# Attention and two MLPs on one core: token sums one a step, an earlier place for the local scores, wide filler products, and a later load

## The chip, the cores and the metric

The program runs on one core of one Trainium2 chip, in fp32 (with fp32r products in the MLPs). The metric is the device time of one execution in microseconds (us). Engines are named as in the profile: PE (TensorE), DVE (VectorE), ACT (ScalarE), POOL (GpSimd) and SP (SyncE, which issues the DMAs).

## What is computed

```python
# q, k, v: (4, 8, 576, 64)
q_d, k_d, v_d = means of q, k, v over groups of 4 positions      # 144 positions
out_up  = repeat(softmax(q_d k_d^T / 8) v_d, 4)
out_loc = softmax(q k^T / 8 where |i - j| < 4) v
x = (out_up + out_loc) as (2304, 512)
x = ((x @ w1) * (x @ w2)) @ w3 @ w_out                           # d_ff 1024
h = x @ w_in;  out = (h * sigmoid(h)) @ w_out2                   # d_ff 2048
```

w3 @ w_out is folded into one matrix while attention runs.

## The kernel before

Attention handles 16 pairs of heads, one pair a **step** (`step(s)`, s = 0 to 15, written once on each engine), and step 16 finishes it. Every engine's order is written out by hand; engines meet in semaphores only. In step s PE does, in this order:

- `scores_down(s)` (L1148): scores of the pooled heads of pair s, read by ACT's exponentials `prob_d`;
- from step 4 on, half of `multiply(q)`, q = s - 4 (L1115): six of the twelve products of one sixteenth of w3 @ w_out; q is called a **half** below, since two of them make a block of 128 rows;
- `turn_local` (L1167) and `turn_down` (L1159): transposes of the probabilities of pair s - 1;
- the other half of `multiply(q)`;
- `scores_local(s+1)` (L1133): banded scores of the next pair, which DVE masks into `sc` (L761) and of which it takes the minimum `low` (L769), which ACT's exponentials (L510) wait for;
- `weighted_local` (L1190) and `weighted_down` (L1177): values of pair s - 1, which DVE adds into `x` (L803) in the step after.

The step of the first transposes is also where steps 1 to 3, which have no `multiply` yet, carry **fillers**: `warm(n)` (L1123) issues products with the identity whose results nobody reads, n by the table `FILL` = (before scores_down, before turn_down, after turn_down).

After every odd q, ACT (L447) and DVE (L735) take the finished bank of w3 @ w_out into `r2` as a high and a low part, at the end of that step; the next q waits for DVE's part. Steps 5, 7, 9, 11, 13 and 15 have such a taking, so steps 6, 8, 10, 12, 14 and 16 have the wait.

DVE's step is: `x` of pair s - 2, maximum of the pooled scores (L775), pooling of the next pair (L749, `qkd`), totals of the exponentials and their inverse (L782 to L788, `inv`), then token sums if the table `TOKENS` has some for the step, then `sc` and `low` of the next pair, the taking of `r2`, and the pooled totals. A **token sum** (L712) is one 128x768 difference of blocks of x, four of them (`tr`), which the first MLP stage reads as one of the operands of a seven-product scheme for 2x2 blocks. POOL multiplies `prob` by `inv` (L424) and takes low parts of w3 (L393).

SP issues the loads in one list: for t = 0 to 15 in the order v (pooled), w3, q and k, v (windows), each with a wait on the engine that frees its buffer. w_out comes in two loads of 1 MB, `load_w_out(0)` and `(1)`; DVE and ACT split them in steps 1 to 5 by `W_OUT`, blocks 4 to 7 (the later half) in steps 3 and 4 on ACT.

After attention come 48 sets of MLP products (L1035, L1064, L1093), which the change does not touch.

Of the kernel before, what the change touches and what calls it, by code (L numbers as in the profile page):

```python
# [12 lines left out]
P = 128  # L13
BANK = 512
# [3 lines left out]
def attention_then_mlps(nc, dims, qk_in, vg_in, vw_in, w3_in, w_out_in, sets_in, w_out2_in, out):  # L18
# [8 lines left out]
    PAIRS = B * HP  # L27
# [58 lines left out]
    with ctx:  # L86
# [3 lines left out]
        def sem(name):  # L90
# [3 lines left out]
        ident = sb("ident", [P, P])  # L94
# [61 lines left out]
        ps = ctx.enter_context(nc.psum_tensor("ps", [P, 8, BANK], F32))  # L156
        pS, pD, pP, pO, pW = 0, 2, 4, 6, 7
# [55 lines left out]


        SUMS = (8, 12)
        TOKENS = {14: (0,), 15: (1, 2, 3)}


        FILL = {1: (30, 4, 2), 2: (6, 6, 2), 3: (6, 6, 2)}
        EXTRA = {8: ("weights", 0), 10: ("tokens", 0), 11: ("weights", 1), 12: ("tokens", 1), 13: ("tokens", 2),  # L220
                 14: ("tokens", 3)}

        def halves_of(s):

# [42 lines left out]
        def _(sp):  # L267
# [47 lines left out]
            for t in range(PAIRS):  # L315
                if t == 1:
                    load_w_out(0)
                    load_qk(3)
                if t + 1 < PAIRS:
                    load_vg(t + 1)  # L320
                if t >= FOLD - 2:
                    load_w3(t - FOLD + 2)
                if t == 1:
                    load_w_out(1)
                if t > 0 and t + 3 < PAIRS:
                    load_qk(t + 3)
                if t + 1 < PAIRS:
                    load_vw(t + 1)
                if t + 2 in SUMS:
                    load_weights(SUMS.index(t + 2))  # L330
# [680 lines left out]
        def _(pe):  # L1011
# [107 lines left out]

            def warm(n):  # L1120

                for _ in range(n):
                    nc.tensor.transpose(ps[:, pW, 0:P], ident[:, :], ident[:, :])  # L1123

            def scores_local(s):
                pe.wait_ge(qk_here[s % 3], 16 * (s // 3) + 16)
# [12 lines left out]
            def step(s):  # L1139
                u, w = s % 2, (s - 1) % 2  # L1140

                def scores_down():
                    pe.wait_ge(pooled, s + 1)
                    after(pe, exp_d, s)
                    for g in range(2):
                        for h in range(2):
                            rows = slice(h * D, (h + 1) * D)
                            e = nc.tensor.matmul(ps[0:PD, pD + h, g * SD:(g + 1) * SD],  # L1148
                                                 qkd[rows, u, 0, g * PD:(g + 1) * PD], qkd[rows, u, 1, :],
                                                 start=True, stop=True)  # L1150
                    e.then_inc(scored, 1)
# [42 lines left out]

                qs = halves_of(s)
                if s == PAIRS:
                    for part in range(2):
                        multiply(qs[0], part)
                    turn_local()
                    turn_down()  # L1200
                    for part in range(2, 4):
                        multiply(qs[0], part)
                    for part in range(2):
                        multiply(qs[1], part)
                    weighted_local()
                    weighted_down()
                    for part in range(2, 4):
                        multiply(qs[1], part)
                    for q in qs[2:]:
                        for part in range(4):  # L1210
                            multiply(q, part)
                    return

                warm(FILL[s][0] if s in FILL else 0)
                scores_down()
                for part in range(2):
                    for q in qs:
                        multiply(q, part)
# [5 lines left out]
                for part in range(2, 4):  # L1224
                    for q in qs:
                        multiply(q, part)
                if s + 1 < PAIRS:
                    scores_local(s + 1)
                if s > 0:
                    weighted_local()  # L1230
                    weighted_down()

            warm(9)
            scores_local(0)
            for s in range(PAIRS + 1):
                step(s)
# [83 lines left out]
```

## Time and profile before

| | us |
|---|---|
| median of 3 runs (lowest, highest) | 804.48 (803.36, 804.74) |
| the profiled execution's own time | 805.16 |
| its span, first to last instruction | 803.3 |
| attention, to the end of the last L1115 | 139.66 |
| PE busy over the span | 783.5 |

The span begins at the first instruction; times in the rows count from there. Attention is the part up to 139.66 us; all that the change touches lies in it.

### The profile page before, as it was taken

The page shows a single profiled execution, that of the slowest core. Times are in us where ns is not written, and L with a number is a line of the kernel's source. Part 1 is how long each engine was busy: PE and PEld are TensorE (multiplying, and loading weights), DVE is VectorE, ACT ScalarE, POOL GpSimd, SP SyncE. Part 2 cuts the span into 40 slices and gives each one's busy share as a digit, 9 for nine tenths or more (in the row PEclk, how much of TensorE's full clock was granted, in tenths as well). Part 3 has the DMA queues.
Part 4 walks back from the last instruction along what each step waited for, and adds up shares of the span by engine and source line. Part 5 has one row for each costly group of instructions (what it writes and reads, how often), then busy time and mean ns, then how long its engine had stood idle before and what let it go on. Part 6 is the DMA issues. An engine that isn't in the chain of part 4 may idle for free.

```text
span 803.3 us, 13951 instructions
## 1 busy us (share of the span) xinstructions
PE 783.5 (98%) x5433; PEld 702.0 (87%) x5433; DVE 587.7 (73%) x939; ACT 347.6 (43%) x791; POOL 272.7 (34%) x305
## 2 busy tenths in 40 slices
PE   7899998999999999999999999999999999999998
PEld 6677776899998999999999888898889888988987
DVE  7887788776678676677778676779677679756644
ACT  6788886422443324332264233254233344433321
POOL 7878985522331331332213221114132113212100
PEclk9899999999999999999999999999999999999999
DMA  9757731111011011011122211223121122312102
GB/s 323 245 184 242 242 125 53 54 53 52 28 53 51 29 53 53 27 53 52 48 84 75 84 53 53 78 80 131 56 101 54 53 79 76 134 53 94 39 1 78
DMA packets 23040, 69.83 MB, mean 87 GB/s; under 512 B 2496, under 2 KB 2496, under 8 KB 22976
## 3 DMA queue, kind: packets, MB, share of 16 engines
q1 hardware_dynamic: 22976, 68.95, 25.5%
q8 instruction: 43, 0.70, 0.3%
q14 instruction: 21, 0.17, 0.1%
HBM read 64.23 MB, written 4.72 MB: 86 GB/s over the span
## 4 chain that ended last, share of the span: by engine, by line
PE 90%; DVE 5%; ACT 3%; issue 1%; DMA 0%; DVEq 0%; ACTq 0%
PE ps L1035 44%; PE ps L1093 25%; PE ps L1064 13%; PE ps L1115 5%; ACT prob L510 1%; DVE sc L761 1%; DVE low L769 1%; PE ps L1133 1%; PE ps L1167 1%; PE ps L1177 1%; PE ps L1190 1%; DVE tr L712 1%; PE ps L1159 1%; DVE qkd L749 0%; PE ps L1148 0%
## 5 line engine op out<-in xcount | busy, mean ns | idle before, releaser
L1035 PE MATMUL ps<-xb,wa 128*128 128x384 f32 x2016 | 404.9, 338 | 0.4 <-DVE mu L863 0.2
L1035 PEld LDWEIGHTS ps<-xb,wa 128*128 128x128 f32 x2016 | 355.1, 188 | 22.4 <-DVE mu L863 1.4
L381 POOL TENSOR_TENSOR rw<-rw 128x256 f32<-128x256 f32 x192 | 170.2, 907 | 448.8 <-DMA rw<-in_sets 336.7
L863 DVE TENSOR_TENSOR mu<-ps,mu 128x384 f32<-128x384 f32 x132 | 73.2, 554 | 123.5 <-PE ps L1035 123.2
L1064 PE MATMUL ps<-g,r 128*128 128x512 f32 (+1 forms) x576 | 124.9, 338 | 2.1 <-issue 2.1
L612 ACT ACTIVATE a<-a 128x384 f32<-128x384 f32 x72 | 37.9, 526 | 187.3 <-DVE a L863 187.3
L1093 PE MATMUL ps<-w2h_even,g 128*128 128x512 f32 x432 | 113.2, 394 | 0.0
L1093 PE MATMUL ps<-w2h_odd,g 128*128 128x512 f32 x432 | 112.5, 393 | 0.0
L718 DVE TENSOR_TENSOR wa<-rw,wa 128x1024 fp32r<-128x1024 f32 x96 | 107.0, 1115 | 3.5 <-ACT wa L447 3.4
L1064 PEld LDWEIGHTS ps<-g,r 128*128 128x128 f32 x576 | 97.7, 188 | 10.6 <-issue 2.6
L1093 PEld LDWEIGHTS ps<-w2h_odd,g 128*128 128x128 f32 x432 | 79.9, 188 | 11.9
L1093 PEld LDWEIGHTS ps<-w2h_even,g 128*128 128x128 f32 x432 | 79.8, 188 | 11.7
L863 DVE TENSOR_TENSOR a<-ps,mu 128x384 f32<-128x384 f32 x108 | 59.9, 555 | 36.6 <-PE ps L1035 35.5
L447 ACT ACTIVATE wa<-rw 128x1792 fp32r<-128x1792 f32 (+2 forms) x49 | 81.4, 1663 | 0.0
L447 ACT ACTIVATE mu<-ps 128x384 f32<-128x384 f32 x48 | 23.4, 487 | 103.5 <-PE ps L1035 103.5
L890 DVE TENSOR_TENSOR g<-a,g 128x384 fp32r<-128x384 f32 x96 | 63.7, 664 | 3.3
L447 ACT ACTIVATE g<-a 128x384 fp32r<-128x384 f32 x48 | 25.2, 526 | 81.8 <-DVE a L869 65.0
L1115 PE MATMUL ps<-r,w3t 128*128 128x512 f32 x192 | 53.4, 418 | 5.9 <-DVE r L735 5.6
L1115 PEld LDWEIGHTS ps<-r,w3t 128*128 128x128 f32 x192 | 35.2, 195 | 15.7 <-issue 8.8
L888 DVE CAST g<-a 128x384 fp32r<-128x384 f32 x96 | 43.7, 455 | 0.0
L510 ACT ACTIVATE prob<-sc,low 128x64 f32<-128x64 f32 x96 | 32.1, 338 | 7.1 <-DVE low L769 6.9
L875 DVE TENSOR_TENSOR g<-a,g 128x384 fp32r<-128x384 f32 x48 | 33.1, 692 | 0.5
(78 smaller groups left out, 705.2 us busy)
## 6 DMA issues: line engine op xcount, KB each, us to landing
rw<-in_sets SPq DMA_DIRECT2D x48, 512.0 KB, 3.5
w2r<-in_w_out SPq DMA_DIRECT2D x24, 512.0 KB, 3.5
qk<-in_qk SPq DMA_DIRECT2D x16, 576.0 KB, 6.6
vg<-in_vg SPq DMA_DIRECT2D x16, 336.0 KB, 4.9
vw<-in_vw SPq DMA_DIRECT2D x16, 320.0 KB, 3.1
out<-osb SPq DMA_DIRECT2D x18, 256.0 KB, 2.5
wn<-in_w SPq DMA_DIRECT2D x16, 256.0 KB, 4.6
raw<-in_w_out SPq DMA_DIRECT2D x2, 1024.0 KB, 12.7
```

The lines of the kernel that those rows point to most:

```text
L381: nc.gpsimd.tensor_tensor(blocks[:, o, :], blocks[:, a, :], blocks[:, b, :], op).then_inc(done, 1)
L447: return nc.scalar.activation(o, a, ACT.Copy)
L510: e = nc.scalar.activation(prob[:, u, g, 1 - h, :], sc[:, g, h, :], ACT.Exp, bias=low[:, u, n:n + 1], scale=-1.0, accum_out=tot[:, u, to, ...
L612: nc.scalar.activation(q, q, ACT.Silu).then_inc(g_act, 1)
L718: e = nc.vector.tensor_tensor(wa[:, k % 2, 1, blocks, :], rw[:, k % 2, 1 + blocks.start:1 + blocks.stop, :], wa[:, k % 2, 0, blocks, :].bi ...
L863: nc.vector.tensor_tensor(o, half_bank(k, i), term, ALU.add).then_inc(sum_ready, 1)
L888: nc.vector.tensor_copy(g[:, 0, j % 2, q // 2, to], a4[:, q, :]).then_inc(g_hi, 1)
L890: nc.vector.tensor_tensor(g[:, 1, j % 2, q // 2, to], a4[:, q, :], g[:, 0, j % 2, q // 2, to].bitcast(F32), ALU.subtract).then_inc(g_lo, 1)
L1035: e = nc.tensor.matmul(ps[:, (k + i) % 2, 0:TH], wa[:, k % 2, l, A_SLOT[i], a * P:(a + 1) * P], xb[:, i, r, a, :], start=(i in (0, 1, 4) a ...
L1064: e = nc.tensor.matmul(o, r2[:, m + MT // 2 * f, l, b * P:(b + 1) * P], g[:, r, n % 2, f, to], start=(first and p == 0 and not (rest and b ...
L1093: e = nc.tensor.matmul(ps[:, 2 + tb, :], g[:, l, j % 2, q // 2, at], w2h[j % 2][:, q // 2, r, :], start=(c == 0 and a < 2 and p == 0), sto ...
L1115: e = nc.tensor.matmul(ps[:, fold_bank(q), :], w3t[:, l, a, :], r3[:, a, r, :], start=(a == 0 and p == 0), stop=(a == MT - 1 and p == 2))
```

## The change

Five edits. The token sums are spread over steps 11 to 14. In steps 5 to 14 `scores_local(s+1)` is issued right behind `scores_down(s)`. `warm(n)` issues plain products of up to 512 columns in place of transposes of 128, and its counts are halved. The later half of w_out is loaded one round of SP's list later. In step 16 the third quarter of q = 12 comes ahead of the transposes. (The table `EXTRA` was read by nothing.)

```diff
--- before.py
+++ after.py
@@ -213,12 +213,10 @@
 
 
         SUMS = (8, 12)
-        TOKENS = {14: (0,), 15: (1, 2, 3)}
-
-
-        FILL = {1: (30, 4, 2), 2: (6, 6, 2), 3: (6, 6, 2)}
-        EXTRA = {8: ("weights", 0), 10: ("tokens", 0), 11: ("weights", 1), 12: ("tokens", 1), 13: ("tokens", 2),
-                 14: ("tokens", 3)}
+        TOKENS = {11: (0,), 12: (1,), 13: (2,), 14: (3,)}
+
+
+        FILL = {1: (15, 2, 1), 2: (3, 3, 1), 3: (3, 3, 1)}
 
         def halves_of(s):
 
@@ -320,7 +318,7 @@
                     load_vg(t + 1)
                 if t >= FOLD - 2:
                     load_w3(t - FOLD + 2)
-                if t == 1:
+                if t == 2:
                     load_w_out(1)
                 if t > 0 and t + 3 < PAIRS:
                     load_qk(t + 3)
@@ -1119,8 +1117,11 @@
 
             def warm(n):
 
-                for _ in range(n):
-                    nc.tensor.transpose(ps[:, pW, 0:P], ident[:, :], ident[:, :])
+                while n > 0:
+                    m = min(n, BANK // P)
+                    nc.tensor.matmul(ps[:, pW, 0:m * P].rearrange("p (m c) -> p m c", m=m), ident[:, :],
+                                     ident[:, None, :].broadcast_to([P, m, P]), start=True, stop=True)
+                    n -= m
 
             def scores_local(s):
                 pe.wait_ge(qk_here[s % 3], 16 * (s // 3) + 16)
@@ -1194,12 +1195,11 @@
 
                 qs = halves_of(s)
                 if s == PAIRS:
-                    for part in range(2):
+                    for part in range(3):
                         multiply(qs[0], part)
                     turn_local()
                     turn_down()
-                    for part in range(2, 4):
-                        multiply(qs[0], part)
+                    multiply(qs[0], 3)
                     for part in range(2):
                         multiply(qs[1], part)
                     weighted_local()
@@ -1213,6 +1213,9 @@
 
                 warm(FILL[s][0] if s in FILL else 0)
                 scores_down()
+                soon = s > FOLD and s + 1 < PAIRS
+                if soon:
+                    scores_local(s + 1)
                 for part in range(2):
                     for q in qs:
                         multiply(q, part)
@@ -1224,13 +1227,13 @@
                 for part in range(2, 4):
                     for q in qs:
                         multiply(q, part)
-                if s + 1 < PAIRS:
+                if s + 1 < PAIRS and not soon:
                     scores_local(s + 1)
                 if s > 0:
                     weighted_local()
                     weighted_down()
 
-            warm(9)
+            warm(4)
             scores_local(0)
             for s in range(PAIRS + 1):
                 step(s)
```

PE in step 5, before. L1148 is scores_down, L1115 multiply, L1167 and L1159 the transposes, L1133 scores_local; the count is of instructions as written, each plain fp32 one of which the trace shows as two.

```order
L1148 MATMUL ps<-qkd 72x144 x4
L1115 MATMUL ps<-r,w3t 128x512 x6
L1167 MATMUL ps<-ident,prob 128x128 x5
L1159 MATMUL ps<-ident,prob_d 112x72 x6
L1115 MATMUL ps<-r,w3t 128x512 x6
L1133 MATMUL ps<-qk 64x64 x20
```

The same place now; lines have moved by up to three, L1134 is scores_local.

```order
L1149 MATMUL ps<-qkd 72x144 x4
L1134 MATMUL ps<-qk 64x64 x20
L1113 MATMUL ps<-r,w3t 128x512 x6
L1168 MATMUL ps<-ident,prob 128x128 x5
L1160 MATMUL ps<-ident,prob_d 112x72 x6
L1113 MATMUL ps<-r,w3t 128x512 x6
```

The twenty local scores have moved ahead of all twelve products of multiply and of the transposes.

DVE in step 15, before, from the pooled maximum on.

```order
L775 TENSOR_REDUCE lowd<-ps 72x2x2
L782 TENSOR_REDUCE tot<-prob 128x4
L786 TENSOR_REDUCE tot<-tot 128x10
L788 RECIPROCAL inv<-tot 128x10
L712 TENSOR_TENSOR tr<-x,tr 128x768
L712 TENSOR_TENSOR tr<-x 128x768
L712 TENSOR_TENSOR tr<-x,tr 128x768
L735 TENSOR_TENSOR r<-ps,r 128x512
```

DVE in step 12 now, where one of them has gone.

```order
L773 TENSOR_REDUCE lowd<-ps 72x2x2
L747 TENSOR_REDUCE qkd<-qk 128x288
L780 TENSOR_REDUCE tot<-prob 128x4
L784 TENSOR_REDUCE tot<-tot 128x10
L786 RECIPROCAL inv<-tot 128x10
L710 TENSOR_TENSOR tr<-x,tr 128x768
L759 SCALAR_TENSOR_TENSOR sc<-ps,mask 128x5x64 x2
L767 TENSOR_REDUCE low<-sc 128x10
```

Three sums have left the way of L735 in step 15, and each of steps 11 to 14 has one ahead of the masking.

PE's first entries, before, to the first turn of the probabilities.

```order
L1123 MATMUL ps<-ident 128x128 x9
L1133 MATMUL ps<-qk 64x64 x20
L1148 MATMUL ps<-qkd 72x144 x4
L1133 MATMUL ps<-qk 64x64 x20
L1123 MATMUL ps<-ident 128x128 x30
```

And now.

```order
L1122 MATMUL ps<-ident 128x512
L1134 MATMUL ps<-qk 64x64 x20
L1149 MATMUL ps<-qkd 72x144 x4
L1134 MATMUL ps<-qk 64x64 x20
L1122 MATMUL ps<-ident 128x512 x3
L1122 MATMUL ps<-ident 128x384
```

Over steps 0 to 3, 73 transposes have become 13 plain products, of about half as many columns in all.

## Rows read from the trace of the kernel before

**Rows 1.** The page: busy time of each engine, its share of the span, instructions.

```profile
PE 783.5 (98%) x5433; PEld 702.0 (87%) x5433; DVE 587.7 (73%) x939; ACT 347.6 (43%) x791; POOL 272.7 (34%) x305
```

**Rows 2.** Stretches of attention: busy us and operations by engine, PE clock, DMA.

```profile
29.60:32.40 2.80, 0.07 (x2) 0.00 (x0) 2.32 (x7) 1.20 (x8) 1.92 (x2) 1.00 0.38 131
32.40:39.60 7.20, 7.18 (x36) 5.30 (x35) 5.22 (x12) 4.95 (x19) 6.12 (x6) 0.53 0.66 214
43.30:86.30 43.00, 41.27 (x718) 31.81 (x716) 35.69 (x78) 37.86 (x167) 37.65 (x39) 1.00 0.69 227
86.30:114.40 28.10, 27.23 (x478) 21.22 (x476) 23.53 (x52) 24.65 (x110) 24.57 (x26) 1.00 0.61 197
...
124.00:128.30 4.30, 4.27 (x18) 3.70 (x19) 4.30 (x6) 1.07 (x3) 4.06 (x4) 0.60 0.13 33
```

**Rows 3.** What PE waited for, 0 to 140 us: total, times, longest.

```profile
PE ps L1115 <- DVE r L735: 5.6, 6, 3.3
PE ps L1190 <- issue: 2.7, 1, 2.7
```

**Rows 4.** Timeline around the pause: start, us, engine, operation, idle before it.

```profile
28.77 0.90 PE L1190 MATMUL ps<-pt,vw 64*64 64x57 f32 x38 [0.18 <-ACT pt L447]
...
32.42 0.27 PE L1190 MATMUL ps<-pt,vw 64*64 64x58 f32 x2 [2.75 <-issue]
...
34.35 0.82 DVE L803 TENSOR_TENSOR x<-ps,od 128x344 f32<-128x344 f32 x2 [1.45 <-ACT od L522]
...
41.98 0.89 DVE L761 SCALAR_TENSOR_TENSOR sc<-ps,mask 128x320 f32<-128x320 f32 x2 [2.72 <-PE ps L1133]
```

**Rows 5.** DMA queues, 29.6 to 31 us: packets, MB, share of 16 engines.

```profile
q8 instruction: 1, 0.02, 4.7%
```

**Rows 6.** The page: instruction queue over the whole span: packets, MB, share.

```profile
q8 instruction: 43, 0.70, 0.3%
```

**Rows 7.** Timeline of PE at step 1, with the first fillers.

```profile
7.61 3.49 PE L1123 MATMUL ps<-ident 128*128 128x128 f32 x30
11.84 0.43 PE L1148 MATMUL ps<-qkd 64*72 64x144 f32 x3 [0.73 <-ACT prob_d L498]
```

**Rows 8.** Timeline of PE, DVE and ACT in steps 13 and 14.

```profile
100.36 0.71 PE L1148 MATMUL ps<-qkd 64*72 64x144 f32 x8
...
104.95 0.81 PE L1133 MATMUL ps<-qk 64*64 64x64 f32 x40
...
105.83 0.89 DVE L761 SCALAR_TENSOR_TENSOR sc<-ps,mask 128x320 f32<-128x320 f32 x2 [1.29 <-PE ps L1133]
...
106.36 0.59 ACT L447 ACTIVATE r<-ps 128x512 fp32r<-128x512 f32 x1
...
107.17 0.71 PE L1148 MATMUL ps<-qkd 64*72 64x144 f32 x8
...
107.49 0.68 DVE L735 TENSOR_TENSOR r<-ps,r 128x512 fp32r<-128x512 f32 x1
...
108.32 1.63 PE L1115 MATMUL ps<-r,w3t 128*128 128x512 f32 x6 [0.43 <-DVE r L735]
```

**Rows 9.** Timeline of step 15 and 16: token sums (L712), POOL, the wait.

```profile
111.86 1.63 DVE L712 TENSOR_TENSOR tr<-x 128x768 f32<-128x768 f32 x1
...
118.48 0.93 DVE L712 TENSOR_TENSOR tr<-x,tr 128x768 f32<-128x768 f32 x1
...
118.67 1.87 POOL L393 TENSOR_TENSOR w3t<-wn,w3t 128x512 fp32r<-128x512 f32 x1
...
119.14 0.60 ACT L447 ACTIVATE r<-ps 128x512 fp32r<-128x512 f32 x1
119.33 2.02 DVE L712 TENSOR_TENSOR tr<-x 128x768 f32<-128x768 f32 x1
...
121.28 2.01 DVE L712 TENSOR_TENSOR tr<-x,tr 128x768 f32<-128x768 f32 x1
...
124.03 2.18 PE L1115 MATMUL ps<-r,w3t 128*128 128x512 f32 x6 [3.30 <-DVE r L735]
```

## The prediction

> **What bounds the kernel now.** I read the page first: PE is busy for 783.5 us, 98% of the span [rows 1], so a change gains by ending PE's waits or a low clock, or by taking work off PE. Then the waits of PE alone in attention. Two kinds stand out: 5.6 us in six waits of L1115 for DVE's `r` (L735), the longest 3.3, and one of 2.75 put down to "issue", that is to nothing that the profile shows [rows 3]. Then the table by stretches, for what such a wait costs afterwards: behind both long idles the granted clock is low, 0.53 over 7.2 us and 0.60 over 4.3 us, where the stretches around have 1.00 [rows 2]; the lower level is 1.2 GHz, the full one 2.4. PE is busy all through these two stretches, so they cost 7.2 x 0.47 = 3.4 and 4.3 x 0.40 = 1.7 us of PE time. Of PE's attention time, then, 2.75 + 3.4 = 6.1 us hang on the pause in step 3, and 3.3 + 1.7 = 5.0 us on the wait for `r` in step 16. Last the timeline of one pair of steps: step 13 goes from 100.36 to 107.17, 6.81 us with no wait in it, and step 14 begins with 0.43 us of idle PE ahead of L1115 [rows 8]. PE's own work of a step is therefore 6.81 us, and what is over that is a wait.
>
> **The change, part by part.**
>
> *Token sums.* In step 15 three sums stand ahead of L735 on DVE. They run from 118.48 to 123.29 [rows 9], 4.8 us. Without them DVE takes `r` as soon as ACT has written its part, at 119.14 + 0.60; with 0.68 for L735 [rows 8] that is 120.4, before PE is through with step 15 at 124.03 - 3.30 = 120.7 [rows 9]. The next operands in the way of PE would be the pair's normalised probabilities: POOL's L424 stood behind one 1.87 us L393 [rows 9], 0.6 of it waiting for a sum, and what follows on POOL comes earlier too; I find them ready in time (an estimate, from the same durations without the stops), with the third quarter of q = 12 put ahead of the transposes (three more products, 0.7 us of cover). So the 3.3 us and the low clock behind it both go: **-5.0 us**.
>
> What do the sums cost where they go? A sum takes 0.93 us alone and 1.63, 2.02 and 2.01 in the other three cases [rows 9]. The third began at 119.33 while POOL's L393 ran until 120.54, and ended 0.81 after that: it stood still until POOL was done. The second ran while L393, begun at 118.67, waited, and took 1.87 for it. One of the two engines stops for the other's whole operation. The Trainium skill says this too (SBUF — State Buffer, Who interferes with whom): a DVE instruction with two SBUF inputs and a GpSimd one that reads SBUF exclude each other, and the second blocks fully; this trace agrees in these rows, and by that rule the moved sums would each tend to the long price, since POOL's L393 and L424 stand at that place in every step. I take 1.3 us as a mean, bounds 0.93 and 2.02. DVE is busy 23.53 us in steps 11 to 14, one sum of 1.63 included [rows 2], so 21.9 without; with four sums 25.6 to 30.0, at 1.3 each 27.1, against 4 x 6.81 = 27.2 of PE. DVE comes close to bound in these four steps and no more, because the earlier scores end DVE's idle 1.29 us ahead of `sc` [rows 8]. PE feels a lag only when `r` is later than the two score blocks that now precede L1115, 1.4 us into a step. I put 0.3 us on steps 11 to 14 for it (bounds 0 and 2.8, the upper from 30.0 - 27.2).
>
> *Local scores earlier.* L1115 of an even step waits for `r`, which waited for ACT at 106.36 + 0.59 and for `sc`, `low` on DVE (105.83 on), which waited for the scores [rows 8]. Now `sc` no longer waits for PE at all, and the scores (L1133, 0.81 us, some 0.75 without overlap [rows 8]) run between scores_down and L1115. ACT's part alone puts `r` at 106.95 + 0.68 = 107.6, and PE wants it at 107.17 + 0.65 + 0.75 = 108.57: the 0.43 us wait is covered. Steps 5 to 10 last 43.0 us [rows 2] against 6 x 6.81 = 40.9, 2.1 over; in step 5 DVE also has w_out's split (L818) and I leave 0.5 of it standing in step 6: **-1.6**. Steps 11 to 15 last 34.4 (86.3 [rows 2] to 120.7) against 4 x 6.81 + 6.1 = 33.3, where step 15 is 6.81 less the scores it does not have. That is -1.1, with the 0.3 above **-0.8**. Nothing is queued badly behind the moved wait: it is for q and k, which land a step earlier, and for `sc` of the pair before, which DVE does in the previous step; if DVE lags by more than a microsecond, scores_local itself will wait there, which is the same lag, not another.
>
> *Fillers.* Thirty transposes take 3.49 us, and PE then still waits 0.73 us for ACT's exponentials [rows 7]. No plain fp32 product of 512 columns is in the trace. Bounds per column and trace entry: 0.62 ns (scores_down, 0.71 us for 8 entries of 144 [rows 8]) and 0.91 ns (a transpose, 3.49 us for 30 of 128 [rows 7]); two entries a product and 1,920 columns give 2.4 to 3.5 us. I take 3.5, since a full 128x128 array is what the transposes have too and the scores not. PE then arrives as before. At 2.4 it would be idle 1.8 us, still under the 2.75 that came ahead of a fallen clock. No time by itself: **0**.
>
> *What the fewer fillers do to the pause.* The pause of 2.75 us falls inside L1190, between its 38th and 39th entry of 40 [rows 4], where the code has no wait. The page has an instruction queue with 43 packets of 16 KB, for 5,433 products and as many weight loads: one block per 253 entries [rows 1, 6]. One of its packets moves between 29.6 and 31 us [rows 5], in the middle of the pause. So I read the pause as PE out of instructions: the block was asked for when the one before was begun, and lay behind data loads. By the counts of the timeline PE had passed 470 products, 940 entries, at the pause. The 73 transposes before it become 26 entries of products (13 of two each), 94 entries fewer with their weight loads; the same block end is now reached in step 4 rather than in step 3, some 5 us later, and its request comes when the queues are nearer to empty (they run low from 30 us on: 38% busy, 131 GB/s in the pause's stretch [rows 2]). The load of w_out that is moved back, 1 MB, leaves the queue ahead of it as long as before at 27 us, and shorter before. It is issued about a step later, and ACT splits it first at the end of step 3, after the pause's place. The Trainium skill (Runtime: NRT & Kernel Launch, Instruction fetch mechanics) has blocks of 256 instructions, fetched through a queue of their own while the current one runs; the rows' 253 agree. It also gives PE room for 2,048 instructions, by which 940 entries could not run dry, and the pause would be of another kind and stay, 797.1: a part of the first rival.
>
> PE gets back up to 6.1 us, but the other engines don't all follow. DVE was idle 1.45 + 2.72 = 4.2 us between the pause and step 5 [rows 4], so its chain can move up by at most 4.2, and it bounds PE at `r` in step 6. POOL and ACT are full in step 4. I take **-3.3** (bounds 0 and -4.2).
>
> *Sum:* -5.0 - 1.6 - 0.8 - 3.3 = -10.7. The rows belong to an execution of 805.16, so 794.5; the median is 0.7 below that execution, so **794.0**. What follows attention moves up whole: its loads and sums wait for PE and DVE's own progress.
>
> **The rivals.**
>
> *The pause stays, or another takes its place.* For it: the request of each block still falls among loads, in steps 5 to 10 the DMA engines are 69% busy [rows 2], and with shorter steps a block has less time; the new place is in step 4. Against: 94 entries are a third of a block, and no later block paused. The gain is then 7.4: 797.1; with a pause in a worse place (the whole 6.1 instead of 3.3), 799.5. Of its chance of 0.2, 0.05 is for a pause that is no lack of instructions and stays at its place.
>
> *DVE becomes the bound in steps 11 to 14.* If every sum takes 2.0, DVE has 30 us of work for 27.2. For it: POOL is 87% busy there (24.57 of 28.1 [rows 2]). Against: POOL's long operations were in the way of three sums in four only, and one engine's stop is then the other's gain. Costs 2.5: 796.5. Chance 0.12.
>
> *Slower.* The one way that I see is that instructions run short again and again: the request now falls just behind SP's batch of loads in every step from 5 on. Each pause costs up to 6.1, so two more than before, with the old one kept, give 7.4 - 12.2 = 4.8 slower, 809; from a second one on it decides. Against it: the waits have a single "issue" entry in all of attention [rows 3], though every step of 5 to 15 used about one block. Chance 0.03.
>
> *The edits do little.* If PE's wait in step 16 is taken over by POOL's L424 and L415, only half of the 5.0 comes back, and with the pause kept too the result is 800 to 803. Chance 0.05.
>
> My forecast has 0.6. Its own range is 792 to 796 (3.3 between 1.5 and 4.2, 0.3 up to 1.5). To leave out no more than 2 in 10 the range takes in the first two rivals: **791 to 799**. Of this kernel a difference below 0.2% (1.6 us) can't be told from none. Faster by more 0.94, within 0.03, slower 0.03.
>
> **What would show it.** The idle of L1115 for `r` near 120 us is gone and the clock stays at 1.00 there; L1115 waits less than 0.3 us in every even step from 8 on; `sc` never waits for PE from step 6 on; the "issue" pause in step 3 is absent, and the clock holds from step 1 to the end of attention; steps 7 to 10 last 6.8 us each; the last L1115 ends near 129 (139.66 before). I am wrong if a pause of over 2 us stands anywhere on PE in attention, if L1115 or scores_local waits for DVE in steps 12 and 14 by more than a microsecond, or if the first scores_down waits longer than before and the clock falls in step 1.

## The result: 798.86 us, faster, with half of the gain that was forecast

| | before | after |
|---|---|---|
| median of 6 runs | 804.54 us (803.36 to 804.90) | 798.86 us (798.22 to 801.34) |
| after / before | | 0.9935, 95% interval 0.9922 to 0.9948 |
| span of the profiled execution | 803.3 us | 796.9 us |
| last L1115 (L1113 after) ends | 139.66 us | 133.07 us |

The kernel is faster by 5.7 us in the medians, and by 5.2 (4.2 to 6.3) by the ratio, which takes in all runs. The forecast was 10.5. The direction was right and the time lies inside the range by 0.1 us, but the gain is about half of what the sum gave. All of the difference lies in attention: from there to the end the two executions take 663.6 and 663.8 us.

The page of the changed kernel, against [rows 1, 6]; the products fell by 47, the 43 blocks of instructions stayed:

```profile
PE 783.3 (98%) x5386; PEld 695.9 (87%) x5386; DVE 591.7 (74%) x939; ACT 347.0 (44%) x791; POOL 272.7 (34%) x305
...
q8 instruction: 43, 0.70, 0.3%
```

What PE waited for between 0 and 142 us (total, times, longest), against [rows 3]:

```profile
PE ps L1113 <- issue: 1.0, 1, 1.0
PE ps L1113 <- DVE w3t L739: 0.7, 1, 0.7
...
PE ps L1113 <- DVE r L733: 0.5, 1, 0.5
PE ps L1113 <- DVE r L816: 0.5, 1, 0.5
```

The two long idles of before are gone: `r` costs 0.5 where it cost 5.6, and there is no "issue" of 2.7 in L1190. Two waits are new, 1.0 and 0.7 us on L1113; the wait of L1168 (L1167 before) for `x` is 1.4 in all where it was 0.6. The stretches (columns as in [rows 2]):

```profile
10.00:30.00 20.00, 18.81 (x340) 12.75 (x338) 18.72 (x39) 18.89 (x87) 16.50 (x17) 1.00 1.01 326
30.00:133.00 103.00, 99.02 (x1504) 74.99 (x1501) 91.11 (x177) 87.46 (x358) 87.56 (x85) 1.00 0.58 184
...
38.92:82.08 43.16, 42.16 (x716) 32.33 (x714) 37.38 (x82) 37.98 (x167) 38.86 (x41) 1.00 0.70 227
82.08:116.80 34.72, 34.49 (x558) 26.22 (x556) 30.97 (x61) 30.34 (x135) 31.84 (x31) 1.00 0.56 176
116.80:133.10 16.30, 14.64 (x111) 11.10 (x110) 14.58 (x17) 11.35 (x23) 9.66 (x8) 1.00 0.22 66
```

The granted clock (third column from the right) is 1.00 in all of attention behind 10 us. In steps 5 to 10 (third row) PE is idle for 1.0 of 43.16 us, in steps 11 to 15 for 0.23, and still these steps are as long as before (43.0 and 34.4). So PE is busy longer with the same products. One step of the timeline shows with what, against [rows 8] (start, us, engine, operation):

```profile
96.01 0.71 PE L1149 MATMUL ps<-qkd 64*72 64x144 f32 x8
96.66 0.81 PE L1134 MATMUL ps<-qk 64*64 64x64 f32 x40
97.40 1.66 PE L1113 MATMUL ps<-r,w3t 128*128 128x512 f32 x6
...
101.34 0.91 PE L1191 MATMUL ps<-pt,vw 64*64 64x57 f32 x40
102.18 0.86 PE L1178 MATMUL ps<-ptd,vd 96*64 96x144 f32 x8
102.97 0.71 PE L1149 MATMUL ps<-qkd 64*72 64x144 f32 x8
```

From start to start scores_local (L1134) takes 0.74 us and weighted_local (L1191) 0.84; before, where they stood behind each other, they took 0.63 and 0.80. From step 7 to step 13 every step lasts 6.96 us, with no wait in it. It remains to look at step 16, PE and DVE:

```profile
122.01 1.48 DVE L716 TENSOR_TENSOR wa<-rw,wa 128x768 fp32r<-128x768 f32 x1
...
123.42 1.48 DVE L728 TENSOR_TENSOR xb<-x,xb 128x768 fp32r<-128x768 f32 x1
...
124.82 1.50 DVE L739 TENSOR_TENSOR w3t<-wn,w3t 128x512 fp32r<-128x512 f32 x1
126.23 1.77 DVE L728 TENSOR_TENSOR xb<-tr,xb 128x768 fp32r<-128x768 f32 x1
126.41 3.00 PE L1113 MATMUL ps<-r,w3t 128*128 128x512 f32 x12 [1.00 <-issue]
127.92 0.81 DVE L801 TENSOR_TENSOR x<-ps,od 128x344 f32<-128x344 f32 x2
128.65 0.68 DVE L733 TENSOR_TENSOR r<-ps,r 128x512 fp32r<-128x512 f32 x1
129.25 0.68 DVE L739 TENSOR_TENSOR w3t<-wn,w3t 128x512 fp32r<-128x512 f32 x1
130.07 3.00 PE L1113 MATMUL ps<-r,w3t 128*128 128x512 f32 x12 [0.66 <-DVE w3t L739]
```

Both new waits end with an L739, the conversion of the low part of w3 on DVE. The first is printed as "issue", but PE goes on 0.09 us after the L739 that began at 124.82 is through. In front of the first, DVE works on L716 and L728, parts that the MLP will need; in front of the second on another L728, on `x` (L801) and on `r` (L733).

The stretches against the forecast's:

| stretch | forecast | measured |
|---|---|---|
| to the start of step 5 (43.32 before, 38.92 after) | -3.3 | -4.4 |
| steps 5 to 10 (43.0 before, 43.16 after) | -1.6 | +0.2 |
| steps 11 to 15 (34.4 before, 34.72 after) | -0.8 | +0.3 |
| step 16, from where PE is ready (120.7 before, 116.80 after) to its last product | -5.0 | -2.7 |

### The profile page after: what moved, and what is told of

The parts are those of the page before. It is cut to its first block, busy times and chain, and to the rows that moved or that the text cites. A ratio compares the mean times of both kernels' runs of the same rounds, so it can differ in the third digit from the quotient of the medians.

```text
span 796.9 us, 13857 instructions
## 1 busy us (share of the span) xinstructions
PE 783.3 (98%) x5386; PEld 695.9 (87%) x5386; DVE 591.7 (74%) x939; ACT 347.0 (44%) x791; POOL 272.7 (34%) x305
## 4 chain that ended last, share of the span: by engine, by line
PE 88%; DVE 9%; ACT 1%; issue 1%; DMA 0%; POOL 0%; DVEq 0%; ACTq 0%
PE ps L1033 44%; PE ps L1091 25%; PE ps L1062 13%; PE ps L1113 2%; DVE qkd L747 1%; DVE sc L759 1%; DVE r L816 1%; DVE low L767 1%; PE ps L1134 1%; DVE tr L710 1%; DVE x L801 1%; PE ps L1191 1%; PE ps L1178 1%; DVE lowd L773 1%; PE ps L1149 0%
## 5 line engine op out<-in xcount | busy, mean ns | idle before, releaser
L716 DVE TENSOR_TENSOR wa<-rw,wa 128x1024 fp32r<-128x1024 f32 x96 | 107.1, 1116 | 3.8 <-ACT wa L445 3.5
L1062 PEld LDWEIGHTS ps<-g,r 128*128 128x128 f32 x576 | 97.8, 188 | 10.5 <-issue 2.6
L1113 PE MATMUL ps<-r,w3t 128*128 128x512 f32 x192 | 52.1, 408 | 2.7 <-issue 1.0
L1113 PEld LDWEIGHTS ps<-r,w3t 128*128 128x128 f32 x192 | 33.7, 188 | 11.3 <-issue 4.0
```

Source lines behind the costliest of these rows:

```text
L716: e = nc.vector.tensor_tensor(wa[:, k % 2, 1, blocks, :], rw[:, k % 2, 1 + blocks.start:1 + blocks.stop, :], wa[:, k % 2, 0, blocks, :].bi ...
L1062: e = nc.tensor.matmul(o, r2[:, m + MT // 2 * f, l, b * P:(b + 1) * P], g[:, r, n % 2, f, to], start=(first and p == 0 and not (rest and b ...
L1113: e = nc.tensor.matmul(ps[:, fold_bank(q), :], w3t[:, l, a, :], r3[:, a, r, :], start=(a == 0 and p == 0), stop=(a == MT - 1 and p == 2))
```

## The experiments

Each is compared with the kernel before on the same chip, whose medians were 804.5, 804.6, 805.8 and 804.7 us on the four chips. Where a run is compared with the changed kernel, that is its median of 798.86 from the result, unless the text says otherwise; what is said of waits and steps comes from one profiled execution of each. Names with b_ are the kernel before with one edit done, names with a_ the changed kernel with one edit undone or altered.

### One edit at a time

**b_fill**: before, with the wide fillers and their counts.

```diff
-        FILL = {1: (30, 4, 2), 2: (6, 6, 2), 3: (6, 6, 2)}
+        FILL = {1: (15, 2, 1), 2: (3, 3, 1), 3: (3, 3, 1)}
...
-                for _ in range(n):
-                    nc.tensor.transpose(ps[:, pW, 0:P], ident[:, :], ident[:, :])
+                while n > 0:
+                    m = min(n, BANK // P)
...
-            warm(9)
+            warm(4)
```

> The kernel before with the wide fillers and their halved counts alone. Theory 1 (the pause in step 3 is PE out of instructions, and 94 entries fewer move the block's end to a later place): the pause of 2.75 us is gone and with it the low clock behind it; the chain through DVE lets 3 to 4 us of it reach the end, 801 us against 804.5. Theory 2 (the pause belongs to its place or to the load of w_out): it stays in L1190 of step 3 and the time is within 0.5 us of before. Both: the wait for r in step 16 stays, 3.3 us, with a low clock behind it.

802.98 us, ratio 0.9977 (0.9966 to 0.9989): 1.5 faster. There is no pause in step 3 any more, and step 5 begins at 38.99 against 43.32. The first theory held for the pause, but not for the time, 801. In the profiled execution the gain is 3.2 us at the start of step 7 (54.87 against 58.10) and 2.5 at the end of attention: the wait for `r` stays at 3.3, and the clock behind it is low for longer than in [rows 2]:

```profile
119.00:125.80 6.80, 5.03 (x19) 4.28 (x20) 6.77 (x9) 2.64 (x5) 4.95 (x6) 0.50 0.20 70
```

**b_tokens**: before, with the new places of the token sums alone.

```diff
-        TOKENS = {14: (0,), 15: (1, 2, 3)}
+        TOKENS = {11: (0,), 12: (1,), 13: (2,), 14: (3,)}
```

> The kernel before with the token sums in steps 11 to 14 alone. Theory 1 (step 16 is bound by DVE's queue of low parts once the 3.3 us wait is gone): PE's wait for r goes, about 1 to 1.7 us of new waits for L741 come in its place, the clock stays full; 2.5 to 3.5 us faster than before, 801.5. Theory 2 (the whole 5.0 comes back and the shortfall of the changed kernel is elsewhere): 799.5. The pause in step 3 stays in both.

803.46 us, ratio 0.9984 (0.9971 to 0.9996): 1.0 faster. The wait of 3.3 is gone and no clock falls behind step 15, but step 14 now lasts 8.11 us instead of 7.28:

```profile
105.93 1.92 DVE L712 TENSOR_TENSOR tr<-x 128x768 f32<-128x768 f32 x1
...
109.41 0.68 DVE L735 TENSOR_TENSOR r<-ps,r 128x512 fp32r<-128x512 f32 x1
110.24 1.63 PE L1115 MATMUL ps<-r,w3t 128*128 128x512 f32 x6 [1.27 <-DVE r L735]
```

A sum stands in front of `sc`, `low` and `r` on DVE, and `sc` had no slack, since its scores came late. L741, the same line as L739 above, costs 0.7 and "issue" 0.5 in step 16 here too. The time is above what either theory gave.

**b_soon**: before, with the early local scores alone.

```diff
+                soon = s > FOLD and s + 1 < PAIRS
+                if soon:
+                    scores_local(s + 1)
...
-                if s + 1 < PAIRS:
+                if s + 1 < PAIRS and not soon:
```

> The kernel before with the early local scores in steps 5 to 14 alone. Theory 1 (0.43 us of wait saved in five steps, 0.15 us lost in ten): steps of 6.96 us each from 7 on, no wait for r in even steps, in all 0.5 to 1.2 us faster, 803.6, with the pause in step 3 and the wait in step 16 as before. Theory 2 (as forecast, steps of 6.81): 802.4.

803.83 us, ratio 0.9987 (0.9974 to 0.9999). From the start of step 5 to that of step 15 it needs 69.90 us where before needs 71.13. The waits for `r` of even steps are gone, and from step 7 on every step lasts 6.96.

Singly the three gain 1.5 + 1.0 + 0.8 = 3.3 us in the medians, and 4.2 by the ratios, each with an interval of some 1 us to both sides; all five edits together gain 5.7, and 5.2 by the ratio. These sums alone don't show that the edits help each other. The steps do: step 14 lasts 8.11 us with the moved sums alone and 7.13 with the early scores beside them. What a term is worth is therefore read below from the kernel with the others in place. The later load and the order of step 16 were not tried alone in the kernel before.

### One edit undone

**a_tokold**: changed, with the token sums at their old places.

```diff
-        TOKENS = {11: (0,), 12: (1,), 13: (2,), 14: (3,)}
+        TOKENS = {14: (0,), 15: (1, 2, 3)}
```

> The changed kernel with the token sums where they were (one in step 14, three in step 15), all else as changed. Theory 1 (moving them is worth the 3.3 us wait and part of the low clock, less 1.7 us of new waits for low parts of w3 in step 16 and less 0.4 of lag in steps 11 to 15): a wait of 3 us or more for r ahead of step 16, a low clock behind it, and 2.5 to 3.5 us over the changed kernel, 801.8. Theory 2 (the sums' move is worth its full 5.0 and the loss is in other edits): 803.8.

802.21 us, ratio 0.9974 (0.9959 to 0.9989): 3.4 slower than the changed kernel. The profiled execution is the fastest of the seven (800.58), and in it attention ends 1.9 later (134.93). The wait and the low clock are back, and the waits for L739 are not there:

```profile
119.34 3.89 PE L1113 MATMUL ps<-r,w3t 128*128 128x512 f32 x9 [3.11 <-DVE r L733]
...
127.83 7.10 PE L1113 MATMUL ps<-r,w3t 128*128 128x512 f32 x30
```

**a_late**: changed, without the early scores.

```diff
-                soon = s > FOLD and s + 1 < PAIRS
+                soon = False
```

> The changed kernel with scores_local(s + 1) behind the multiplies in every step again, so without the early local scores; all else as changed. Theory A, the term of my forecast (-1.6 in steps 5 to 10 and -0.8 in steps 11 to 15): 798.9 + 2.4 = 801.3; steps 7 to 11 alternate between 6.81 and 7.28 us instead of 6.96, and in steps 11 to 14, where DVE has the token sums and would stop again for the scores, they last 7.3 or more. Theory B: early scores gain only what they gained alone (804.6 to 803.8, 0.8 us), since each early block costs PE 0.15 us in the weighted_local that now stands behind a 512-column product: 799.7. Above 800.5 A, below 800.2 B.

801.24 us, ratio 0.995 (0.9933 to 0.9968): 2.4 slower (2.6 against a_quarter on the same chip, which is no different from the changed kernel). L1113 has five waits for `r`, 3.2 us in all, steps 7 to 10 alternate between 6.8 and 7.3, and step 14 takes 8.10 as in b_tokens. Step 15 begins at 112.16 instead of 110.10. My term of 2.4 holds, though alone the edit gains 0.8: it is the slack that it gives DVE that lets the token sums stand in steps 11 to 14.

**a_narrow**: changed, with the filler transposes and counts of before (the diff of b_fill the other way).

> The changed kernel with the transposes of before as fillers (73, and the old counts), all else as changed. Theory 1 (entry count decides): a pause of 2 to 3 us is back in step 3 near the 940th entry, the clock falls behind it, and the time is 3 to 4 us over the changed kernel, 802.5. Theory 2 (the later load of w_out removed the pause): no pause, time as the changed kernel, 798.9.

799.96 us, ratio 0.9936 (0.9921 to 0.9951). **a_wout**: changed, with the later half of w_out at its old place.

```diff
-                if t == 2:
+                if t == 1:
                     load_w_out(1)
```

> The changed kernel with the later half of w_out loaded where it was before, all else as changed. Theory 1 (the fillers alone moved the pause, the load's place is nearly free): within 0.5 us of the changed kernel, no pause. Theory 2 (the load decides): a pause of over 1 us and 3 to 4 us more, 802.5.

799.12 us, ratio 0.993 (0.9913 to 0.9946). Both times can't be told from the changed kernel's, and neither profile has the pause. My reading had put all of it on the count of fillers, and that fell here: with the old count and the later load there is no pause either. In a_wout a wait of 2.0 us for x in step 3 had half the clock behind it, for 3.4 us:

```profile
27.70:31.10 3.40, 3.40 (x23) 2.45 (x24) 3.40 (x4) 2.79 (x11) 3.24 (x4) 0.50 0.82 245
```

**a_both**: changed, with both of these edits undone; beside it **a_anchor**, the changed kernel as it is.

> The changed kernel with both early edits undone: the narrow filler transposes with their old counts, and the later half of w_out at its old place (t == 1). So token sums, early local scores and the order of step 16 alone. Theory (a shortage of instructions that needs both the old entry count and that load in the way, since either edit undone alone showed no pause): the pause is back in step 3, after the 472nd product, 2 to 4 us long, and the clock is low behind it. The end of attention in the profile is then 3 to 4.5 us later than in the changed kernel, as my term of -3.3 says: 801.5 to 803. Rival: the term is worth what the wide fillers gained alone, 1.5 us, since the engines behind PE give part of the pause back: 800.4.

> The changed kernel as it is, on the same chip as the run beside it, since the median of the kernel before was 1.2 us higher in one call than in the others. If that was the chip, the changed kernel comes out 5.7 us under its kernel before, between 798 and 800, with the two waits for w3_low (1.00 and 0.66 us) in step 16.

a_anchor 798.72 us (0.9921, 0.9904 to 0.9938); a_both 801.27 (799.83 to 803.16; 0.9954, 0.9937 to 0.9972), 2.6 slower. (On this chip the changed kernel gains 6.0 us in the medians.) The pause is back at its place, between the 38th and the 39th product. The profiled execution is the fastest of the seven and shows a short one, of 1.77 us, with no low clock behind it:

```profile
29.63 0.87 PE L1188 MATMUL ps<-pt,vw 64*64 64x58 f32 x38
32.27 0.27 PE L1188 MATMUL ps<-pt,vw 64*64 64x58 f32 x2 [1.77 <-issue]
```

A second, of 1.3 us, stands in step 4 on L1175. So, in these four kernels, the pause needs the old count of entries and that load in the queue.

### What the pause is

**b_shift**: before, with two more fillers at the very start.

```diff
-            warm(9)
+            warm(11)
```

> The kernel before with two more filler transposes at the very start (warm(11) for warm(9)): with their weight loads four trace entries more ahead of everything. Theory (a block of the program's code arrives late, and PE has run out of instructions): the pause of 2.7 us stays in step 3 but falls two products earlier in weighted_local, between its 36th and 37th entry instead of the 38th and 39th, at the same count of entries from the start; about 805. Rival (a wait or a port in weighted_local itself, or a place in the code): the pause stays between the 38th and 39th, or is somewhere else.

```profile
29.85 0.75 PE L1190 MATMUL ps<-pt,vw 64*64 64x58 f32 x36
32.49 0.33 PE L1190 MATMUL ps<-pt,vw 64*64 64x58 f32 x4 [1.89 <-issue]
...
50.01 0.71 PE L1148 MATMUL ps<-qkd 64*72 64x144 f32 x8 [0.69 <-issue]
```

Two more products at the start, and the pause falls two products earlier in a block of 40 that has no wait in it. The stretches up to the two idles (PE's count is the first in brackets):

```profile
0.00:32.00 32.00, 24.57 (x472) 20.61 (x473) 25.50 (x47) 23.69 (x106) 23.00 (x37) 1.00 0.92 307
0.00:49.60 49.60, 41.37 (x722) 33.04 (x722) 41.72 (x78) 37.92 (x166) 37.48 (x50) 0.97 0.79 261
```

It is 472 products in the kernel before too, and in b_tokens, b_soon and a_both. The second idle comes 250 products later, 500 entries with their weight loads, which is two blocks by the 253 of [rows 1, 6]. So a pause is bound to a count of instructions, not to a place in the work. (One execution, 804.0 us.) The 944 entries themselves are no whole number of such blocks; instructions that the trace doesn't count would have to make up the rest.

The traces show more than that: when the instruction queue's one packet moves ahead of each pause, and when PE goes on (us, read to 0.05).

| kernel | packet moves | PE goes on | between |
|---|---|---|---|
| before | 29.85 | 32.42 | 2.6 |
| b_tokens | 30.80 | 33.21 | 2.4 |
| b_soon | 31.75 | 34.26 | 2.5 |
| b_shift | 29.80, 47.60 | 32.49, 50.01 | 2.7, 2.4 |
| a_both | 29.90, 38.50 | 32.27, 41.01 | 2.4, 2.5 |

PE goes on 2.4 to 2.7 us behind the packet in all seven, whether it has stood still for 0.7 us or for 3.7. That fits a lack of instructions. It also says why one edit is enough. In a_both PE is through with its 472nd product at 30.50; the packet moves at 29.90, and 2.4 us behind it is 32.3, too late by 1.8. In a_narrow, with the later load, PE is as far at about the same time, but the packet has moved at 26.00. In a_wout, with fewer entries, the packet moves at 29.85 as before, but PE gets to its 472nd product only behind 37.98. That the load of w_out is what holds the packet up by those 4 us is argued from this one pair.

### Step 16 and the length of a step

**a_w3**: changed, with DVE's order in step 16 altered; the token parts and the last x are moved behind the conversions of w3.

```diff
+            w3_low(HALVES - 2)
             tokens_low(0, 0)
-            w3_low(HALVES - 2)
+            take_w3o(MT - 2)
+            w3_low(HALVES - 1)
             tokens_low(0, 1)
             take_local(PAIRS - 1)
-            take_w3o(MT - 2)
-            w3_low(HALVES - 1)
```

> The changed kernel with DVE's order in step 16 turned so that the low parts of the last two halves of w3 (L739) come ahead of the token parts (L728) and of the last x. Theory 1 (PE's two waits of 1.0 and 0.66 us there are DVE's queue): both go, 1.2 to 1.7 us faster than the changed kernel, 797.4. Theory 2 (the halves wait for the load of w3 or for ACT, or the products behind wait for the token parts instead): waits of the same sum stand there or at L1033, and the time is within 0.4 us of 798.9.

797.87 us, ratio 0.9913 (0.9899 to 0.9927), 1.0 faster than the changed kernel in the median of four runs, with intervals that overlap; the profile is what shows the effect. PE has no wait at all in step 16, and the last 30 products run in one piece:

```profile
125.07 7.15 PE L1113 MATMUL ps<-r,w3t 128*128 128x512 f32 x30
```

Behind the waits they took 1.66 + 3.00 + 3.00 = 7.66 us in three pieces: each stop cost, beside its own length, 0.25 us. I take that for a pipeline that ran empty, which was not tried. Step 16 goes from 118.11 to 132.22, 14.1 us against 16.3, so 2.2 back. The median shows 1.0 of it; in this profiled execution 1.3 was lost earlier, for another reason (last section). Step 16 begins 1.3 us later here than in the changed kernel, but that is not why the waits are gone: in a_wout and a_both it begins at 118.12, and both waits are there, 1.00 and 0.65 to 0.68 us.

**a_even**: changed, with early scores in even steps only.

```diff
-                soon = s > FOLD and s + 1 < PAIRS
+                soon = s > FOLD and s % 2 == 0 and s + 1 < PAIRS
```

> The changed kernel with the local scores behind the pooled ones in even steps only (6, 8, 10, 12, 14), in odd ones at their old place. Theory 1 (the early place costs 0.15 us in every step, since the weighted sums then stand behind a product of another shape instead of behind the scores): odd steps last 6.82, even ones 6.96 us or little more, 0.5 to 0.9 us faster, 798.2. Theory 2 (the 0.15 us is DVE's or ACT's lag): odd steps stay at 6.96 or grow, since the scores of the next pair come later again, and the time is 0.5 us or more above 798.9.

799.74 us, ratio 0.9939 (0.9925 to 0.9953), no gain. But it puts both orders side by side in one kernel, step 7 with the scores behind the multiplies and step 8 with them ahead:

```profile
58.88 0.81 PE L1134 MATMUL ps<-qk 64*64 64x64 f32 x40
59.52 0.87 PE L1191 MATMUL ps<-pt,vw 64*64 64x58 f32 x40
60.32 0.86 PE L1178 MATMUL ps<-ptd,vd 96*64 96x144 f32 x8
...
61.75 0.81 PE L1134 MATMUL ps<-qk 64*64 64x64 f32 x40
62.49 1.65 PE L1113 MATMUL ps<-r,w3t 128*128 128x512 f32 x6
...
66.44 0.91 PE L1191 MATMUL ps<-pt,vw 64*64 64x57 f32 x40
67.28 0.86 PE L1178 MATMUL ps<-ptd,vd 96*64 96x144 f32 x8
```

Behind each other the two blocks of 40 take 60.32 - 58.88 = 1.44 us. Apart they take 0.74 + 0.84 = 1.58. Steps 7 to 12 alternate between 6.81 and 6.96. From step 7 on this had won 0.47 us by the start of step 13 (95.61 against 96.01, from 54.30 against 54.23), and by step 15 it was gone, which begins at 110.32 (110.10 in the changed kernel): steps 13 and 14 last 7.20 and 7.51.

**a_best**: a_w3 with the scores early in even steps up to 10 and in all from 11 on.

```diff
-                soon = s > FOLD and s + 1 < PAIRS
+                soon = s > FOLD and (s % 2 == 0 or s > 10) and s + 1 < PAIRS
```

> The changed kernel with w3_low of the last two halves ahead of the token parts and of the last x on DVE in step 16 (as in the run that has only this), and the local scores early in even steps up to 10, and in every step from 11 on. Theory: in odd steps 5, 7 and 9 the scores stay behind the multiplies, weighted_local then takes 0.69 and not 0.84 us, and those steps last 6.81 us instead of 6.96; 3 x 0.15 = 0.45 below the run with the order in step 16 alone, 797.4, with steps 12 and 14 at 6.96 and no wait of PE for DVE in step 16. Rival: DVE bounds these steps, since it would stop for PE in odd steps, and what PE saves is waited off in step 11 or 12: 797.9, no different.

798.09 us, ratio 0.991 (0.9893 to 0.9926): no different from a_w3, and again without a wait in step 16. Step 14 lasts 7.58, with 0.59 us of L1113 waiting for `r`. The rival held: what PE saves, it waits off behind DVE.

**a_quarter**: changed, with the third quarter of the first multiply of step 16 behind the transposes again.

```diff
-                    for part in range(3):
+                    for part in range(2):
                         multiply(qs[0], part)
                     turn_local()
                     turn_down()
-                    multiply(qs[0], 3)
+                    for part in range(2, 4):
+                        multiply(qs[0], part)
```

> The changed kernel with the third quarter of the first multiply of step 16 behind the two transposes again. My forecast counted three products, 0.7 us, as cover for the turned local probabilities. Theory A: the cover is needed, turn_local waits for x or for POOL and ACT 0.5 to 0.7 us in step 16: 799.4. Theory B: nothing is late there, PE's waits in step 16 are for w3_low (L739) only, and they stay 1.66 us: 798.9, no different.

798.65 us, ratio 0.9922 (0.9906 to 0.9938), the same as the anchor's. The cover that I had counted was not needed: of the two waits of step 16 the one put down to "issue" is 0.5 long, the one for L739 0.7 as before.

## Why the forecast was half right

**Right.** The bound, PE's two long idles and the clock behind them; both went, and the clock holds to the end of attention. The pause as a lack of instructions, a reading that b_shift and the packets bear out: the 472nd product is its place whatever stands there. By the Trainium skill (Runtime: NRT & Kernel Launch, Instruction fetch mechanics) blocks of 256 are fetched ahead, and PE has room for 2,048. The blocks agree with the trace, 500 entries for two. No use of such a room shows: PE stood still at its 944th entry, for a packet that had moved 2.6 us before. The price of the fillers: 3.5 us was forecast for those of step 1, and a_anchor takes 3.49 (the profile of the changed kernel 4.18, see Open). The early scores: `sc` never waits for PE, and the term of 2.4 was 2.4 with the other edits in place. The price of the token sums, mean 1.3 us between 0.93 and 2.02, came out so:

```profile
86.03 0.94 DVE L710 TENSOR_TENSOR tr<-x 128x768 f32<-128x768 f32 x1
93.24 1.63 DVE L710 TENSOR_TENSOR tr<-x,tr 128x768 f32<-128x768 f32 x1
100.21 1.94 DVE L710 TENSOR_TENSOR tr<-x 128x768 f32<-128x768 f32 x1
108.09 1.63 DVE L710 TENSOR_TENSOR tr<-x,tr 128x768 f32<-128x768 f32 x1
```

Their mean is 1.5, and PE was not kept back until the last: step 14 lasts 7.13, and behind the sum at 108.09 `low` begins at 110.55, so that ACT's exponentials come late and step 15 takes 6.70 us. With the sums at their old places (a_tokold) it takes 6.29.

**The step that failed: "So the 3.3 us and the low clock behind it both go: -5.0".** They go, but not the whole time comes back: what is late now is w3_low (L739, L741 before) of the last two halves. I had followed the chain of `r` and POOL's L424, and no further down DVE's queue. In the kernel before the conversion for q = 14 was ready at 131.72, and PE wanted it at about 134.1, 1.5 us into its last thirty products:

```profile
123.21 0.68 DVE L735 TENSOR_TENSOR r<-ps,r 128x512 fp32r<-128x512 f32 x1
...
131.04 0.68 DVE L741 TENSOR_TENSOR w3t<-wn,w3t 128x512 fp32r<-128x512 f32 x1
...
132.56 7.10 PE L1115 MATMUL ps<-r,w3t 128*128 128x512 f32 x30
```

From the end of `r` (123.89) that is 7.8 us for DVE and 10.2 for PE, 2.3 to spare. In the changed kernel `r` ends at 116.60. DVE needs 9.7 us from there (to 126.32), and PE wants the same conversion after 8.7 (at about 125.3), 1.0 too early. Three things changed. PE's products took 10.0 us from the first of step 16 to q = 14 behind the fallen clock, and take 8.5 now. While PE stood still and DVE was at its sums, ACT got through its exponentials `prob_d` (L498, to 121.4); now DVE waits for them behind `r`:

```profile
117.57 0.16 DVE L791 TENSOR_REDUCE totd<-totd 72x4 f32<-72x8 f32 x1 [0.97 <-ACT prob_d L496]
```

And the L739 itself takes 1.50 us instead of 0.68; POOL's L435 runs from 124.04 to 127.18 beside it, where the same operation began behind that conversion before (L437, 131.91). Whether that is the reason was not tried. The wait and the slow clock had been cover for all of this. The two stops are 1.66 us and what they cost beside 0.5: 2.2 of the 2.3 us that were missing in step 16. a_w3 shows it by taking them away. In medians the term is 3.4 (a_tokold), not 5.0.

**The second: "PE's own work of a step is therefore 6.81 us".** It was that in the old order. An edit that puts scores_local elsewhere splits two like blocks, and the step is 6.96. In steps 5 to 14 that is 10 x 0.15 = 1.5 us, 0.9 of it in steps 5 to 10 and 0.6 in steps 11 to 14. In steps 5 to 10 there come 0.9 more, since step 5 lasts 7.83 us and step 6 7.48, with waits of 0.46 for DVE's L816 and 0.47 for its `r`, and I had left only 0.5 for both: 1.8 in all. In steps 11 to 15 another 0.17 in step 14 and 0.41 in step 15 come on top for DVE's lag, for which I had 0.3, and 0.19 because step 15 without scores takes 6.29 us and not the 6.1 of my sum: 1.07 of the 1.1 missing.

**The third: "I take -3.3".** In medians the term measured 2.6 in company and 1.5 alone. In the profile step 5 begins 4.4 us earlier, and steps 5 and 6 give 0.9 of that back, which leaves 3.5: DVE bounds PE there, as I had said. The mechanism was more than I had said: I gave the count of fillers as its cause and the load of w_out as a help, and either edit alone is enough to end it. The pause is 1.8 to 3.7 us long in the five kernels that have it, so one profiled execution gives no good mean of it.

What the four stretches are short of the forecast is -1.1 + 1.8 + 1.1 + 2.3 = 4.1 us in the profiled executions. The medians lie another 0.7 closer together than these do (6.4 in span, 5.7 in medians). That the time fell inside the range is partly luck: the range had been widened for two rivals, a pause and DVE as the bound of steps 11 to 14, and neither is what happened. Nearest came the rival that the edits do little: half of the 5.0 did stay away, but through DVE's L739 and not through POOL's L424. Two sums of the prediction have a slip: 805.16 - 10.7 - 0.7 is 793.8 and not 794.0, and a pause in a worse place comes to 799.9 and not 799.5. Neither changes the outcome.

Open: why PE's first products are slow in the profile of the changed kernel. L1149 takes 1.24 us at 5.91 and L1134 1.35 at 7.08, 0.71 and 0.81 before, and the rows print a clock of 1.00 there. It is not the fillers alone: a_narrow, with the nine old ones at the start, shows the same 1.24 and 1.35. Step 3 begins at 24.65 against 24.58, so by then it has cost nothing.

## What to carry to other kernels

A wait of several microseconds on the bounding engine, with a slow stretch behind it, is cover for every queue that it takes work from. Before it is counted as a gain, go through the whole queue of the other engines up to the next thing that the bounding engine takes from them, and give each the new, earlier time at which it is wanted; work that is wanted only later belongs behind that.

The cost of a block of small products depends on what stands ahead of it, so a reordering has a price even where it adds nothing. Edits that give slack and edits that use it must be tried together: the moved sums made step 14 last 8.11 us alone and 7.13 beside the early scores.

## What the runs showed of the hardware

Two blocks of 40 small products took 1.44 us behind each other and 1.58 with the 512-column products between them (a_even), with the same products otherwise.

An idle of PE put down to "issue" in a block without waits can be counted: it stands behind the same product (the 472nd) in five kernels, and others stand 250 (b_shift) and 125 (a_both) products on, and one of 0.22 us 125 ahead (b_soon). PE went on 2.4 to 2.7 us behind the packet of the instruction queue.

The pair of L816 on DVE in step 2 can take either time in kernels with the same code up to there. First the changed kernel, then a_w3, with the operation that POOL had begun 0.12 us before:

```profile
19.82 2.26 POOL L402 TENSOR_TENSOR vt<-vg 112x384 f32<-112x384 f32 x1
19.94 1.28 DVE L816 TENSOR_TENSOR r<-raw,r 128x512 fp32r<-128x512 f32 x2
```

```profile
19.99 1.00 POOL L402 TENSOR_TENSOR vt<-vg 112x384 f32<-112x384 f32 x1
20.11 2.44 DVE L816 TENSOR_TENSOR r<-raw,r 128x512 fp32r<-128x512 f32 x2
```

One of the two stands still for the other: where DVE is short, POOL is long by 1.26 us, and where POOL is short, DVE is long by 1.16. a_anchor is like the first and a_quarter like the second. The Trainium skill (SBUF — State Buffer, Who interferes with whom) says that such a DVE instruction and a GpSimd one exclude each other, and these rows agree. What decides who goes first does not show in them: both begin 0.12 us apart, in the same order.

DVE is busy through these steps, and what follows moves by as much: x in step 3 is waited for 1.9 us instead of 0.75, and step 4 starts at 32.13 instead of 31.12. A profile in which a start differs by 0.2 us can so differ by one a little later, and a difference of 1 us in one execution says nothing yet.
